# Shorter token steps in a recurrence followed by a two-layer product: 448 tokens per step in place of 512

## The reference

```python
sig = 1 / (1 + exp(-f_logit));  f = lb + (1 - lb) * sig;  i = 1 - f
for t in range(S):                       # S = 6080
    h = f[:, t] * h + i[:, t] * x[:, t]
    y[:, t] = h
a = y.reshape(12160, 256) @ w_in         # 256 -> 2048
g = a * clip(a + 3, 0, 6) / 6
out = g @ w_out                          # 2048 -> 256
```

## Time and profile before

| | |
|---|---|
| median of 3 runs | 1084.76 us (1084.72 to 1084.92) |
| span of the profiled execution, first to last instruction | 1083.2 us |
| what the median has beyond that span | 1.6 us |
| PE busy | 1074.5 us |
| PE weight loads busy | 873.8 us |
| DVE busy | 621.4 us |
| ACT busy | 533.2 us |
| POOL busy | 70.9 us |
| matmuls | 4636 (28 of them the warm-up) |
| moved by DMA | 41.74 MB, mean 39 GB/s |

### The profile page before, as it was taken

One profiled execution on the slowest core, in us unless ns is written; L12 is line 12 of the kernel. 1 busy time (PEld: TensorE's weight loads), 2 busy tenths in 40 slices (PEclk: granted clock), 3 DMA queues, 4 the chain that ended last, 5 costly groups with the idle time before them and its releaser, 6 DMA issues.

```text
span 1083.2 us, 12791 instructions
## 1 busy us (share of the span) xinstructions
PE 1074.5 (99%) x4636; PEld 873.8 (81%) x4636; DVE 621.4 (57%) x950; ACT 533.2 (49%) x859; POOL 70.9 (7%) x37
## 2 busy tenths in 40 slices
PE   7999999999999999999999999999999999999998
PEld 7998888888888888888888888888888888888886
DVE  7865564655646556465564655646556465564644
ACT  5655454454544545444454444544445445454443
POOL 3300000000000000000000000000000000000000
PEclk9999999999999999999999999999999999999999
DMA  7011010110101101011010110101101001010000
GB/s 262 1 56 56 1 59 0 58 58 0 58 6 52 58 0 58 13 46 58 0 58 17 41 58 0 58 21 37 58 0 58 24 34 58 0 58 20 1 20 19
DMA packets 22093, 41.74 MB, mean 39 GB/s; under 512 B 1600, under 2 KB 3136, under 8 KB 22080
## 3 DMA queue, kind: packets, MB, share of 16 engines
q1 hardware_dynamic: 22080, 41.56, 11.4%
HBM read 29.10 MB, written 12.45 MB: 38 GB/s over the span
## 4 chain that ended last, share of the span: by engine, by line
PE 98%; DVE 0%; ACT 0%; issue 0%; ACTq 0%
PE y_ps L465 49%; PE h_ps L445 49%; DVE state L349 0%; DVE state_lo L379 0%; ACT clipped L263 0%; DVE g_lo L364 0%; DVE g L359 0%; DVE drive L342 0%; ACT y_sb L324 0%; ACT state_hi L277 0%; ACT g_hi L268 0%; ACTq L262 0%
## 5 line engine op out<-in xcount | busy, mean ns | idle before, releaser
L263 ACT ACTIVATE clipped<-h_ps,half 128x512 f32<-128x512 f32 (+1 forms) x384 | 263.2, 686 | 533.6 <-PE h_ps L445 533.6
L359 DVE SCALAR_TENSOR_TENSOR g<-clipped,h_ps 128x512 f32<-128x512 f32 (+1 forms) x384 | 261.7, 682 | 450.2 <-ACT clipped L263 450.1
L445 PE MATMUL h_ps<-state_hi,w_in_hi 128*128 128x512 f32 (+1 forms) x768 | 303.2, 395 | 3.3 <-DVE state_lo L379 3.3
L465 PE MATMUL y_ps<-g_hi,w_out_hi 128*128 128x512 f32 (+1 forms) x768 | 302.5, 394 | 1.0 <-DVE g_lo L364 1.0
L445 PE MATMUL h_ps<-state_lo,w_in_hi 128*128 128x512 f32 (+1 forms) x768 | 302.8, 394 | 0.0
L445 PE MATMUL h_ps<-state_hi,w_in_lo 128*128 128x512 f32 (+1 forms) x768 | 302.7, 394 | 0.0
L465 PE MATMUL y_ps<-g_lo,w_out_hi 128*128 128x512 f32 (+1 forms) x768 | 302.3, 394 | 0.0
L465 PE MATMUL y_ps<-g_hi,w_out_lo 128*128 128x512 f32 (+1 forms) x768 | 302.3, 394 | 0.0
L364 DVE TENSOR_TENSOR g_lo<-g,g_hi 128x512 fp32r<-128x512 f32 (+1 forms) x384 | 271.2, 706 | 0.2
L268 ACT CAST g_hi<-g 128x512 fp32r<-128x512 f32 (+1 forms) x384 | 233.0, 607 | 1.6 <-DVE g L359 1.4
L445 PEld LDWEIGHTS h_ps<-state_hi,w_in_hi 128*128 128x128 f32 x768 | 144.9, 189 | 37.0 <-DVE state_lo L379 2.9
(11 more groups left out here) (23 smaller groups left out, 77.9 us busy)
## 6 DMA issues: line engine op xcount, KB each, us to landing
z_sb<-in_z SPq DMA_DIRECT2D x22, 512.0 KB, 4.5
x_sb<-in_x SPq DMA_DIRECT2D x22, 512.0 KB, 5.1
out_y<-y_sb SPq DMA_DIRECT2D x21, 512.0 KB, 3.3
w_in_raw<-in_w_in SPq DMA_DIRECT2D x8, 256.0 KB, 5.9
w_out_raw<-in_w_out SPq DMA_DIRECT2D x8, 256.0 KB, 7.1
out_y<-y_sb SPq DMA_DIRECT2D x2, 448.0 KB, 3.5
out_y<-y_sb SPq DMA_DIRECT2D x2, 256.0 KB, 2.1
z_sb<-in_z SPq DMA_DIRECT2D x2, 224.0 KB, 3.7
```

The costliest lines, as they stand in the source:

```text
L263: nc.scalar.activation(clipped[:, s, 0:n], h_ps[:, s, 0:n], ACT.Relu, bias=half[:], scale=1.0 / 6.0).then_inc(clipped_ready, 1)
L359: nc.vector.scalar_tensor_tensor(g[:, s, 0:n], clipped[:, s, 0:n], 1.0, h_ps[:, s, 0:n], ALU.min, ALU.mult).then_inc(g_ready, 1)
L445: last = nc.tensor.matmul(h_ps[:, s, 0:n], w[:, f, k, :], v[:, b, k, 0:n], start=(k == 0 and m == 0), stop=(k == K - 1 and m == len(terms) ...
L465: last = nc.tensor.matmul(y_ps[:, b, d, 0:n], w[:, f, at], v[:, s, 0:n], start=(f == 0 and m == 0), stop=(f == F - 1 and m == len(terms) - 1))
```

## The change

The step is 448 tokens in place of 512. 6080 = 13 x 448 + 256, so there are 14 steps, the first of 256 tokens: 28 tiles, the first two of 256 and 26 of 448. The buffers keep rows of 512 words, so each row begins where it did before. The copy at the end of the last tile names its columns, since the rows are now longer than N. All else follows from N.

```diff
-N = 512
+N = 448
+ROW = 512
...
-        x_sb = sb("x_sb", [P, B, K, N])
-        z_sb = sb("z_sb", [P, B, K, N])
+        x_sb = sb("x_sb", [P, B, K, ROW])
+        z_sb = sb("z_sb", [P, B, K, ROW])
...
-        state_hi = sb("state_hi", [P, B, K, N], F32R)
+        state_hi = sb("state_hi", [P, B, K, ROW], F32R)
...
-        g_hi = sb("g_hi", [P, SLOTS, N], F32R)
+        g_hi = sb("g_hi", [P, SLOTS, ROW], F32R)
...
-            nc.vector.tensor_copy(y_sb[:, B - 1, 0], y_ps[:, B - 1, 0]).then_inc(y_head_copied, 1)
+            nc.vector.tensor_copy(y_sb[:, B - 1, 0, 0:N], y_ps[:, B - 1, 0, 0:N]).then_inc(y_head_copied, 1)
```

More of the change, by code:

```diff
@@ L83, in build @@
         warm = sb("warm", [P, WARM_N], F32R)
-        x_sb = sb("x_sb", [P, B, K, N])
-        z_sb = sb("z_sb", [P, B, K, N])
[L87 to L90, removed]
-        carry = sb("carry", [P, B, K])
-        state_hi = sb("state_hi", [P, B, K, N], F32R)
-        state_lo = sb("state_lo", [P, B, K, N], F32R)
-        clipped = sb("clipped", [P, SLOTS, N])
-        g = sb("g", [P, SLOTS, N])
-        g_hi = sb("g_hi", [P, SLOTS, N], F32R)
-        g_lo = sb("g_lo", [P, SLOTS, N], F32R)
-        y_sb = sb("y_sb", [P, B, K, N])
+        x_sb = sb("x_sb", [P, B, K, ROW])
+        z_sb = sb("z_sb", [P, B, K, ROW])
+        sig = sb("sig", [P, K, ROW])
+        gate = sb("gate", [P, K, ROW])
+        drive = sb("drive", [P, K, ROW])
+        state = sb("state", [P, K, ROW])
+        carry = sb("carry", [P, B, K])
+        state_hi = sb("state_hi", [P, B, K, ROW], F32R)
+        state_lo = sb("state_lo", [P, B, K, ROW], F32R)
+        clipped = sb("clipped", [P, SLOTS, ROW])
+        g = sb("g", [P, SLOTS, ROW])
+        g_hi = sb("g_hi", [P, SLOTS, ROW], F32R)
+        g_lo = sb("g_lo", [P, SLOTS, ROW], F32R)
+        y_sb = sb("y_sb", [P, B, K, ROW])
         h_ps = ctx.enter_context(nc.psum_tensor("h_ps", [P, SLOTS, 512], F32))
```

## The result

The forecast was 1065.6 us (1062 to 1070). Measured: **1099.76 us** (1099.21 to 1100.16, 4 runs) against 1084.74 (1084.52 to 1084.92, 4 runs); ratio **1.0135** [1.0121, 1.015]. The change made the kernel 1.35% slower where I forecast 1.8% faster. The profiled execution has a span of 1097.9 us, 1.9 under the median.

A forecast was written before the change was run, and what follows sets the result against it. PE was taken as the bound: number of matmuls times start-to-start distance. Terms -20.1 - 3.2 + 0.3 + 3.2 + 0.8 - 0.2 = -19.2 us gave a span of 1064.0, median 1065.6 us (1062 to 1070).

The forecast's parts named there:

- The steady part: All matmuls but the 24 ahead of the first `down`: 1061.7 us before, 1041.6 after, with 448 columns at 0.200; -20.1 us.
- So it is the width: Claim that width, not neighbours or loop, sets the matmul distance: 0.2000 us at 448 columns, 0.2343 at 512.
- Until the first `down`: Start-up latency chain with 192 columns fewer per operation: first `down` at 14.6 us, -3.2 us (bounds -1.9 and -3.9).
- The brake that I named: Before the first `down`: POOL's two `w_in_lo` and a `w_out_lo` of unchanged size; if not earlier, first `down` at 15.3.
- The clock term: At the start, PE idles more and may run another stretch at half clock: +0.3 us (0 to 1.5).
- Tile 0: Fixed weight work against half the PE cover, with waits for `g_lo` and POOL: +3.2 us (bounds +1 and +6).
- Tile 1: No weights, but DVE prepares the 448-column tile 2, 9.5 us against 7.2 of PE: +0.8 us (0 to 2).
- The end: Copy and store after PE's last matmul, at 448 columns: -0.2 us.
- B: Rival: in the loop 448 columns also pay 21.0 ns over the columns, 207.6 ns; +35 us, 1101 us; 3%.
- C: Rival: a fixed surplus of 13.3 ns at every width, so 768 added matmuls cost 10.2 us; 1096 us; 2%.
- A: Rival: the start-up gives nothing to the small tiles, tile 0 paced by weights as before; +12.6, 1078 us; 6%.
- D: Rival: the clock stays at half through tile 0, 18 us less 3.6 of covered waits; 1080 us; 2%.

## Why the prediction was wrong, by its steps

**The steady part: the step that failed.** I wrote "26 x 192 = 4992 at 0.200 = 998.4", on the ground that "it is the width". The width was right in so far as 448 can be had at 200.0; what was wrong is that a width has *one* price. The stream measured 206.7, which is 33.1 us more over the 4968 matmuls from tile 2's first `down` on. With the pace forced to 200.0 by one cut, the same kernel takes 1066.51 us against a forecast of 1065.6 (span 1064.2 against 1064.0). The evidence lay in the trace of before, about ten matmuls behind a wait at 39.64 us, and tile 0 itself was 0.4 us too long, which I put down to the wait alone. I counted one clean stretch and took its exactness (200.0 throughout) for proof.

**"So it is the width", from both widths side by side**: that argument was weaker than it looked. The 0.20 from 86.44 to 86.64 lies ahead of the first 512-column matmul, at the end of the pure stream. The next `down`, at 88.04 us between groups of 512, has distances of 205, 208, 203, 201, 200 and 200 ns, so 448 columns did not cost 200.0 wherever they stood. And a mixed stream cannot show what a pure one settles to.

**Until the first `down`.** Forecast 14.6 us, measured 14.70. The brake that I named, POOL, did not bind: its `w_out_lo` ended at 12.37 us (before, 15.15), and PE's wait ended with DVE's `g_lo` at 14.55. The clock term (+0.3) did not arise. The first real matmul followed the warm-up at once, at 7.33 us; PE then idled three times for 1.2, 1.2 and 1.8 us, and behind each the distances were soon at 115 to 124 ns again, the higher level, where before six distances of 0.37 us (448 columns at 1.2 GHz, granted clock 0.50) followed soon behind an idle 2.68 us. Why no such stretch came is not shown. The granted clock reads 1.00 over all the first 14.7 us, but the warm-up's matmuls were 213 ns apart until 7 us, which is 256 columns at 1.2 GHz: over the warm-up that column cannot be read as speed.

**Tile 0.** Forecast 26.2 us, measured 27.2, with waits for `g_lo` and for POOL's `w_out_lo` as forecast. They lay ahead of `down` 1, 6, 8 and 10 (0.4 to 1.1 us each); ahead of 4 and 9, which I had named too, they were 0.2 us or less. The waits after, from 14 to 68 us (total, times, longest):

```profile
PE y_ps L466 <- DVE g_lo L365: 5.4, 6, 1.7
...
PEld y_ps L466 <- POOL w_out_lo L226: 2.0, 3, 1.0
```

A wait of PE and that of its weight load overlap, so they don't add. The narrow matmuls were a little cheaper than my 0.120, which I had read off six starts of the warm-up: six in 0.71 us in the chain of after, 0.118.

```profile
37.65 0.71 PE y_ps L466 x6
```

**Tile 1.** Forecast 25.8, measured 26.0 (41.90 to 67.93), with one long wait, ahead of `down(9)`. The stream began at 67.93 us; my three parts add to 66.6, but they leave out the clock's 0.3, and 26.2 for tile 0 takes off the 0.4 of before twice. By the sum itself all but the stream had 1064.0 - 993.6 = 70.4 us (4968 x 0.200 = 993.6); measured are 1097.9 - 1026.7 = 71.2 (4968 x 0.20667). That is 0.8 more, and with the stream's 33.1 it makes the 33.9. **The end**: as forecast; the copy after PE's last is 0.53 us.

**The rivals.** B gave 1101 us, near to what came, but for a reason that is refuted: it held the loop responsible, and the straight code of tiles 26 and 27 runs at the same 206.7, and the last `up` of tile 1, ahead of the loop, has distances of 203 to 207 ns. It had 3%. C, a fixed surplus, is out: surpluses over columns / 2.4 GHz were 10.7 or 12.0 ns at 256, 13.3 at 320 (first tiles of the 480-token run, 146.7 ns), 13.3 or 20.0 at 448, 16.7 or 17.8 at 480, 21.0 at 512. The rule in the Trainium skill, "TensorE: Matmul & The Clock Gate", section "Wait — 56ns, not 53.3ns?", columns over 2.4 GHz plus about 2.5 ns, would be 189 ns at 448; no stream of this kernel ran so. A and D did not happen.

**Which pace is entered** is known in part. Where the stream opens straight out of tile 1's mix of 256 and 448 columns, with no wait, it repeats to the nanosecond. In the changed kernel and in the runs with 40 warm-up matmuls, with rows of 448 words, and with one cut a tile at 320 and at 256, the distances in the last `up` ahead of the stream are 203, 206, 207, 207, 206, 207 ns, and the stream goes on at 206.7; that fits the four runs of the changed kernel lying within 1 us. Behind a wait it does not repeat. In tile 0 the wait ahead of `down(9)` led to 206.7 in the kernel before and to 200.0 in the same code of two other runs (512 with cuts; short step last). The first `down` led to 200.0 in the run with the short step last (first distance 280 ns) and to 206.7 in the same code of the run that adds the cuts at 320 (282 ns).

**Still open.** What in the hardware makes two paces, and the rule by which a wait, a cut or a mix of widths leads to one or the other; none was tried. Streams without a weight load for each matmul, and other operand types, were not tried.

## What to carry to other kernels

Where PE is the bound and its stream never stops, its pace can be one of several, set by what goes just before the stream and kept to its end. Before you price a width, list the distances in every stretch of the trace, above all behind waits, and treat a second value as a second pace, with a chance of its own. If a stream sits in the slower pace, one matmul cut in two in front of it (here at column 320 of 448) can move it, at a cost of tens of nanoseconds; column 384 did not move it, and 256 moved it either way. A steady number read over one stretch is exact for that stretch only.

## What the runs showed of the hardware

The distance of a stream of weight load and matmul pairs, per column: 256 columns 0.458 or 0.463 ns, 448 columns 0.4464 or 0.4613, 480 columns 0.4514 or 0.4538, 512 columns 0.4576. The two at 256 come from the 256-token tiles at the end: 117.3 ns in the run with the short step last (1050 to 1080 us), 118.7 ns in the one that adds the cuts at 320 (1020 to 1050 us). The same 448-column stream kept either pace for over 900 us, through loop ends and tile ends, beside DMA and all engines. A cut at column 256 swapped the two paces every time, 384 kept whichever it met, 224 kept 200.0, 320 led to 200.0 from both.
